# A network on one core: the back product's first wait asks for eleven low halves instead of twelve, and a four-instruction fold is issued in three steps

## The reference, cut to what matters

```python
def _moe_ref(x, w_ch1, w_ch2):             # x: 4 x 768 x 384
    X = np.fft.fft(x, axis=1)
    X = np.fft.fft(X, axis=2)
    mixed = np.real(X).astype(np.float32)
    u = x + mixed
    mu = np.mean(u, axis=-1, keepdims=True)
    var = np.mean((u - mu) ** 2, axis=-1, keepdims=True)
    un = (u - mu) / np.sqrt(var + 1e-06)
    ch = np.maximum(un @ w_ch1, 0.0) @ w_ch2   # 384 -> 1536 -> 384
    return (u + ch).astype(np.float32)
```

## Time and profile before

| what | value |
|---|---|
| median of three runs | 835.82 us |
| the profiled execution, its own time | 835.56 us |
| its span | 833.7 us |
| TensorE (PE) busy | 776.8 us, 93% of the span |
| VectorE (DVE) busy | 519.4 us, 62% |
| ScalarE (ACT) busy | 317.7 us, 38% |
| GpSimd (POOL) busy | 164.6 us, 20% |
| chain that ended last: PE, DVE, waiting for nothing seen, ACT | 82%, 8%, 4%, 3% |

### The profile page before, as it was taken

How to read it: one execution, slowest core, us unless ns; L and a number is a source line. 1 busy time by engine, 2 the same in 40 slices (tenths; PEclk the granted TensorE clock), 3 DMA queues, 4 the chain that set the end, 5 groups by cost and what they waited for, 6 DMA issues and landing times.

```text
span 833.7 us, 24886 instructions
## 1 busy us (share of the span) xinstructions
PE 776.8 (93%) x10976; PEld 546.9 (66%) x10976; DVE 519.4 (62%) x1238; ACT 317.7 (38%) x635; POOL 164.6 (20%) x201
## 2 busy tenths in 40 slices
PE   4699889898789999999999999999999999999998
PEld 3588888787777556555656566656566666666664
DVE  4998979787847783724472346365646767757422
ACT  3466555555542350403141224142432534524211
POOL 2542332322200102200130010003122323323100
PEclk9699999999999999999999999999999999999999
DMA  9143333322121141010101000000000000000101
GB/s 208 45 95 94 92 89 90 88 71 61 42 80 42 57 132 39 6 53 0 32 28 57 0 30 29 1 0 2 0 1 2 11 20 20 29 14 26 39 25 52
DMA packets 45389, 37.54 MB, mean 45 GB/s; under 512 B 27424, under 2 KB 39650, under 8 KB 45282
## 3 DMA queue, kind: packets, MB, share of 16 engines
q1 hardware_dynamic: 38501, 30.90, 13.1%
q10 hardware_dynamic: 6781, 5.05, 2.4%
HBM read 26.50 MB, written 4.72 MB: 37 GB/s over the span
## 4 chain that ended last, share of the span: by engine, by line
PE 82%; DVE 8%; issue 4%; ACT 3%; DMA 1%; SPq 0%; POOL 0%; DVEq 0%; ACTq 0%
PE bank L305 14%; PE bank L1081 6%; PE bank L1129 6%; PE bank L1083 6%; PE bank L1128 6%; PE bank L1127 6%; PE bank L1082 6%; PE bank L1065 5%; PE bank L1067 5%; PE bank L1066 5%; PE bank L337 2%; PE bank L1004 2%; PE bank L1000 1%; PE bank L360 1%; PE bank L1105 1%
## 5 line engine op out<-in xcount | busy, mean ns | idle before, releaser
L1246 ACT ACTIVATE hT_hi<-bank 128x384 f16<-128x384 f32 x96 | 46.6, 489 | 162.7 <-PE bank L1067 162.6
L1520 DVE SCALAR_TENSOR_TENSOR hT_lo<-bank,hT_hi 128x384 f16<-128x384 f32 x96 | 53.3, 556 | 73.5 <-ACT hT_hi L1246 72.9
L1065 PE MATMUL bank<-unT,wA 128*128 128x384 f16 x288 | 94.0, 326 | 2.1 <-DVE hT_lo L1520 2.1
L1081 PE MATMUL bank<-wA,hT_hi 128*128 128x384 f16 x288 | 94.1, 327 | 1.3 <-DVE hT_lo L1520 1.3
L1067 PE MATMUL bank<-unT,wA 128*128 128x384 f16 x288 | 93.9, 326 | 0.0
L1066 PE MATMUL bank<-unT,wA 128*128 128x384 f16 x288 | 93.9, 326 | 0.0
L1083 PE MATMUL bank<-wA,hT_lo 128*128 128x384 f16 x288 | 93.9, 326 | 0.0
L1082 PE MATMUL bank<-wA,hT_hi 128*128 128x384 f16 x288 | 93.9, 326 | 0.0
L305 PE MATMUL bank<-Yv,ET 64*64 64x48 f32 x2304 | 75.3, 218 | 5.6 <-issue 3.0
L305 PEld LDWEIGHTS bank<-Yv,ET 64*64 64x64 f32 x2304 | 72.7, 135 | 8.5 <-ACT Yv L443 4.5
L443 ACT ACTIVATE Yv<-bank,rows 128x384 f32<-128x384 f32 x72 | 40.6, 578 | 67.2 <-PE bank L305 67.1
(11 more groups left out here) (212 smaller groups left out, 1658.6 us busy)
## 6 DMA issues: line engine op xcount, KB each, us to landing
Kb<-k_dram SPq DMA_DIRECT2D x24, 192.0 KB, 3.5
Vv<-v_dram SPq DMA_DIRECT2D x12, 384.0 KB, 3.8
z_first<-w_dram SPq DMA_DIRECT2D x8, 576.0 KB, 4.1
z_first<-wt_dram SPq DMA_DIRECT2D x8, 576.0 KB, 3.6
out_dram<-hT_hi SPq DMA_DIRECT2D x24, 192.0 KB, 1.9
KQ<-q_dram SPq DMA_DIRECT2D x44, 96.0 KB, 2.3
X<-Yo ACTq DMA_DIRECT2D x12, 192.0 KB
X<-Yo ACTq DMA_DIRECT2D x10, 189.0 KB
```

The source lines that it names most:

```text
L1065: pe.matmul(out, w1[0][:, k, cols], unT[0][:, k, :], start=(k == 0), stop=False)
L1081: pe.matmul(out, hT[0][:, f, cols], w2[0][:, f, :], start=(f == 0), stop=False)
L1246: act.activation(hT[0][:, f, :], bank[3 + m % 3][:, 0:TG * P], ACT.Relu).then_inc(s_hh, 1)
L1520: dve.scalar_tensor_tensor(hT[1][:, f, :], bank[3 + m % 3][:, 0:TG * P], 0.0, hT[0][:, f, :], ALU.max, ALU.subtract).then_inc(s_hl, 1)
```

## The change

`back(n, 0)` now waits for eleven low halves before its first matmul, and for the twelfth before the first matmul that reads tile 11. `even_fold` takes a list of steps, and the vector block issues step 0 (the sum of token tiles) after tile 5, step 1 (the fold) after tile 10 and step 2 (the two parts) after tile 11. The calls ahead of the loop issue all three steps at once as before.

```diff
             def back(n, i):
                 m = TG * n + i
                 if i == 0:
-                    pe.wait_ge(s_hl, KF * (n + 1))
+                    pe.wait_ge(s_hl, KF * n + KF - 1)
                 if m >= 2:
                     pe.wait_ge(s_x2, m - 1)
...
                 for f in range(KF):
                     if m == 0 and f % KD == 0:
                         pe.wait_ge(s_wd, W2 + f // KD + 1)
+                    if i == 0 and f == KF - 1:
+                        pe.wait_ge(s_hl, KF * (n + 1))
                     pe.matmul(out, hT[0][:, f, cols], w2[0][:, f, :], start=(f == 0), stop=False)
...
-            def even_fold(b, js):
+            def even_fold(b, js, steps=range(3)):
                 x = xe[:, js]
+                if 0 in steps:
+                    even_added(b, js, x)
+                if 1 in steps:
+                    dve.wait_ge(s_xe, b + 1)
+                    dve.tensor_tensor(x[:, :, 1:DH - 1], x[:, :, 1:DH - 1], x[:, :, DM - 1:DH - 1:-1], ALU.add).then_inc(s_xe2, 1)
+                if 2 in steps:
+                    dve.wait_ge(s_xe2, b + 1)
+                    even_parts(b, js, s_fold)
+
+            def even_added(b, js, x):
                 if b:
                     dve.wait_ge(s_fold, 2 * b)
                 if b >= 2:
                     dve.wait_ge(s_st1, 4 * (b - 1))
                 dve.tensor_tensor(x, X[:, 2 * js.start:2 * js.stop:2, b, :], X[:, 2 * js.start + 1:2 * js.stop:2, b, :],
                                   ALU.add).then_inc(s_xe, 1)
-                dve.wait_ge(s_xe, b + 1)
-                dve.tensor_tensor(x[:, :, 1:DH - 1], x[:, :, 1:DH - 1], x[:, :, DM - 1:DH - 1:-1], ALU.add).then_inc(s_xe2, 1)
-                dve.wait_ge(s_xe2, b + 1)
-                even_parts(b, js, s_fold)
...
-                    if n in (1, 3) and f == 6:
-                        even_fold(b + 2, slice(0, NJ))
+                    if n in (1, 3) and f in (5, 10, 11):
+                        even_fold(b + 2, slice(0, NJ), ((5, 10, 11).index(f),))
```

## The result

The changed kernel takes 830.84 us, the median of nine runs (827.4 to 834.42), against 835.82 for nine of the kernel before on the same chip: a ratio of 0.9939, with a 95% interval of 0.9921 to 0.9957. The forecast was 831.2, from a sum of 4.6 us saved.

What follows compares the result with a forecast made beforehand. TensorE's list of work and its standstills were taken to bound the kernel from the eight groups on; 1.92 (fold) + 2.71 (wait) = 4.63 us off the profiled 835.56 gave 830.9, forecast 831.2 us, range 829.9 to 833.7.

Steps and rivals of the forecast that it cites:

- Rival 4: Third layer: TensorE arrives earlier but waits for something else, at the angles or mixing; no difference, 835.8 us; chance 0.04.
- Rivals 1 and 2: Only the fold pays, 833.9 us, chance 0.05; or only the back product's wait pays, 833.1 us, chance 0.05.
- The fold, 1.92: Hidden tile 10, groups 1 and 3: splitting the fold removes two stalls of 0.95 us, 1.92 us in all.
- Tile 9's cover of 1.26 us: Group 1: tile 6's low half ends at 341.91, TensorE wants it for tile 9 at 343.17, 1.26 us later.
- The 0.22 ahead of tile 11: Fold's second step, behind tile 10, was to end 0.22 us before tile 11's low half starts.
- The wait, 2.71: Start of back(n, 0): asking for eleven halves saves 2.22 us in groups 0 to 5, with groups 6 and 7 2.71.
- The new wait in the middle, 0: Ahead of matmul 34 of 36 in eight back products: taken as 0, at most 0.08 us in all.
- rival 5: Even a met wait in mid back product makes TensorE drain what it loaded ahead; slower, 838.8 us; chance 0.02.
- The port: VectorE's two-input SBUF instructions and GpSimd's SBUF reads exclude each other; no meeting expected, the sum starting 1.24 us behind GpSimd's fold.
- rival 3: Fold's sum meets a 2.62 us GpSimd instruction, two stalls at tile 9, 0.8 us more; 833.9 us; chance 0.02.
- about 0.5 us in two waits left at L1065: Hidden products: TensorE's waits for low halves were to fall from 2.1 us to about 0.5.
- The span of 829.1: Whole profiled trace after the change: its span was to be 829.1 us.

Runs made afterwards that it cites:

- e1: Kernel before with only the back product's new wait, the fold whole after tile 6 as before; ratio to the kernel before 0.9973.
- e2: Kernel before with only the fold split after tiles 5, 10 and 11, the old wait kept; ratio to the kernel before 0.9971.
- e3: Changed kernel with the whole fold after tile 5; first hidden matmul to end, without group 0's standstills, 539.51 us against 538.77.
- e6: Changed kernel with a wait ahead of every hidden tile of back(n, 0); first hidden matmul to end, without group 0's standstills, 538.79 us against 538.77.
- e7: Changed kernel with the fold's first sum after tile 2, beside GpSimd's fold; first hidden matmul to end, without group 0's standstills, 538.90 us, 0.13 more.
- e4: Changed kernel with the whole fold after tile 10; first hidden matmul to end, without group 0's standstills, 538.78 us against 538.77.
- e5: As e4, but the back product waits for all twelve halves at its start; first hidden matmul to end, without group 0's standstills, 546.98 us.

## Why the prediction was right

- **What bounds.** TensorE's list, from the first hidden matmul on. What was cut from its standstills came off the end undiminished: 4.60 us of 4.63. Rival 4, that it would be given back in the third layer, falls: that layer takes 210.0 us before and after. Rivals 1 and 2 fall with e1 and e2, each half having paid what was forecast for it.
- **The fold, 1.92.** Measured alone: 1.91. The covers were read right where it counts. At tile 6 the half was to be 0.39 late and was 0.28 late. Tile 9's cover of 1.26 us is confirmed by e3, which overdraws it by 0.34 to the 0.4 reckoned. The 0.22 ahead of tile 11 was 0.24.
- **The wait, 2.71.** Measured alone: 2.68. Taking distances between starts made this term: by the idle times of the earlier trace rows it would have been 1.3.
- **The new wait in the middle, 0.** With ten more like it per group (e6), no more than 0.02 us for all 80, so rival 5 falls.
- **The port.** No meeting in the changed kernel; where one is forced (e7), it is real, and cost TensorE 0.13 us, not the 0.8 of rival 3, since it met a shorter GpSimd instruction (1.40 us instead of 2.62) in a place whose cover was overdrawn by only 0.05.
- **What was off.** The forecast of about 0.5 us in two waits left at L1065; the changed kernel's trace has 0.3 in one, its repeat 0.5 in two, and e2 0.8, since they hang on the landing of weights. The span of 829.1 forecast for the trace: it was 826.6, by 2.4 us ahead of the first hidden matmul, not by this change. That the median came within 0.4 us of the forecast is partly luck, since the nine times lie up to 7 us apart; the sum is borne out by the yardstick. The sum rested on two places where the fold stood, and didn't see that the new wait alone would have let the fold stand whole after tile 10.

## What to carry to other kernels

Where one engine is the bound, list its standstills by the distance between starts, not by the idle time that a modelled end leaves, and ask of each wait which instruction reads what it waits for: a wait at the first of 36 matmuls for what the 34th reads costs 0.37 us here at six of the eight starts, and 80 more waits that are met cost nothing that could be measured. When a side job of another engine is moved, reckon for each place the time from its end to the moment at which the bound engine wants what is queued behind it; in e3, e4 and e5 each standstill came out within about 0.1 us of that reckoning, and what it missed is the fall of the clock in e5. A change of half a per cent is verified on the stretch that it touches, against a repeat of both kernels.

## What the runs showed of the hardware that was not expected

- What lies ahead of the first hidden matmul is the same program in all thirteen traces, and yet that matmul starts between 287.2 and 296.4 us (two executions of the changed kernel: 287.2 and 295.4), while from there on two executions agree within 0.01 us once the weights' landing is taken out. Of the 8.5 us between the spans of the changed kernel's two traces, 8.2 lie ahead of it. Half-rate stretches of TensorE's granted clock and "issue" waits (those for which the profile shows no cause) differ between the executions there; which of them makes the 9 us wasn't tried.
- In e5 the granted clock fell after one standstill of 2.28 us and not after another of the same length 87 us earlier (0.59 in the 4.2 us behind the one, 1.00 in the 5.4 us behind the other).
- VectorE and GpSimd, where one waited for the other in e7, show it in the duration of their rows and not as idle time: 2.25 instead of 1.35 us, 1.47 instead of 0.34.
